# Routing constants made later, and a tile's row copy ahead of the addition to the counts

## The reference, cut

```python
q_pool = q.reshape(B, H, S // 2, 2, D).mean(axis=3)
attn = softmax(scale * q_pool @ k.T)             # scale = 1 / sqrt(D)
x = (attn @ v)                                   # as tokens: N = 2304 rows, 512 columns

# first layer of experts (8 experts, 512 -> 1024 -> 512)
do_compute = x @ w_skip > 0                      # the others keep x
e_idx = argmax(x @ w_gate);  gate_w = probability of that expert
x = x + gate_w * (relu(x @ w1[e_idx]) @ w2[e_idx])

# second layer
e_idx = argmax(x @ w_gate2); gate_w = its probability
eom = sigmoid(x @ w_output_gate)
out = gate_w * eom[e_idx] * (relu(x @ w1b[e_idx]) @ w2b[e_idx])
```

## Time and profile before

| | us |
|---|---|
| median of 3 runs | 1131.06 |
| lowest and highest | 1129.37, 1131.52 |
| the profiled execution | 1127.29 |
| its span, first to last instruction | 1125.5 |
| attention, to the last head's sums | about 549 |
| first layer's tiles | about 571 to 796 |
| change to the second layer | about 796 to 814 |
| second layer | 814 to the end |

### The profile page before, as it was taken

The page is one execution under the profiler, slowest core; times in us unless marked ns, Lnnn a source line. Parts: engine busy times, 40 slices in busy tenths (PEclk is TensorE's granted clock), DMA queues, the critical chain, the costliest instruction groups (busy, mean ns, idle before and its releaser), DMA issues.

```text
span 1125.5 us, 22186 instructions
## 1 busy us (share of the span) xinstructions
PE 1092.2 (97%) x7849; PEld 921.4 (82%) x7849; DVE 741.0 (66%) x1706; ACT 531.8 (47%) x945; POOL 459.0 (41%) x337
## 2 busy tenths in 40 slices
PE   7999999999999999999799999999899999999996
PEld 5777777777777777777598999999799999999995
DVE  7767767887778877786446777777465655566641
ACT  3566655655555665554225444444054344254320
POOL 0768877777876788777600000000000101111100
PEclk9999999999999999999899999999899999999999
DMA  5273225223322233311659014447385281231100
GB/s 132 66 232 75 64 75 149 72 70 95 104 65 74 75 86 96 81 37 33 231 177 354 28 38 179 165 182 277 127 336 175 75 328 37 78 138 40 44 10 15
DMA packets 74398, 132.61 MB, mean 118 GB/s; under 512 B 11040, under 2 KB 29472, under 8 KB 74320
## 3 DMA queue, kind: packets, MB, share of 16 engines
q1 hardware_dynamic: 43568, 50.84, 16.9%
q10 hardware_dynamic: 26096, 68.96, 16.7%
q0 software_dynamic: 4656, 11.79, 3.0%
HBM read 106.12 MB, written 19.24 MB: 111 GB/s over the span
## 4 chain that ended last, share of the span: by engine, by line
PE 94%; DVE 2%; issue 1%; ACTq 1%; ACT 0%; SPq 0%; DMA 0%; POOL 0%; DVEq 0%; POOLq 0%
PE PS L765 24%; PE PS L600 14%; PE PS L514 11%; PE PS L566 9%; PE PS L573 8%; PE PS L583 7%; PE PS L778 6%; PE PS L782 6%; PE PS L779 6%; PE PS L615 1%; PE PS L638 1%; PE PS L797 1%; DVE mx L1070 1%; ACTq L846 0%; DMA moe<-xs 0%
## 5 line engine op out<-in xcount | busy, mean ns | idle before, releaser
L454 POOL TENSOR_TENSOR arena_a<-arena_a,arena_p 128x576 f32<-128x576 f32 x222 | 330.3, 1488 | 85.3 <-ACT arena_p L883 62.7
L1070 DVE TENSOR_REDUCE mx<-PS 128x1 f32<-128x384 f32 (+1 forms) x480 | 246.3, 551 | 108.9 <-PE PS L566 105.3
L765 PE MATMUL PS<-moe,W 128*128 128x128 f32 x2432 | 279.0, 276 | 1.5 <-ACT moe L969 1.5
L765 PEld LDWEIGHTS PS<-moe,W 128*128 128x128 f32 x2432 | 276.2, 192 | 3.7 <-ACT moe L969 1.9
L883 ACT ACTIVATE arena_p<-PS 128x576 f32<-128x576 f32 x288 | 187.6, 653 | 132.0 <-PE PS L583 131.5
L573 PE MATMUL PS<-QHT,KA 128*128 128x288 f32 x576 | 182.0, 329 | 0.0
L1175 DVE TENSOR_TENSOR W2L<-W2R,W2H 128x1024 fp32r<-128x1024 f32 x144 | 169.8, 1220 | 16.4 <-ACT W2H L855 15.9
L566 PE MATMUL PS<-KA,QHT 128*128 128x384 f32 (+1 forms) x480 | 173.7, 364 | 2.2 <-DVE mx L1070 2.0
L583 PE MATMUL PS<-QLT,KB 65*128 65x288 f32 x576 | 171.1, 301 | 0.2 <-ACT QLT L894 0.2
L855 ACT CAST W2H<-W2R 128x1024 fp32r<-128x1024 f32 x148 | 144.3, 1048 | 50.4 <-PE PS L782 41.6
L600 PE MATMUL PS<-arena_p,arena_a 128*64 128x288 f32 x1152 | 160.5, 414 | 0.0
(11 more groups left out here) (181 smaller groups left out, 1154.1 us busy)
## 6 DMA issues: line engine op xcount, KB each, us to landing
W<-in_moe_w ACTq DMA_DIRECT2D x16, 2048.0 KB, 14.9
W2R<-in_moe_w ACTq DMA_DIRECT2D x16, 2048.0 KB, 9.8
moe<-xs SPq DMA_DIRECT2D x40, 258.0 KB, 2.7
arena_a<-in_k SPq DMA_DIRECT2D x32, 288.0 KB, 3.0
arena_a<-in_v SPq DMA_DIRECT2D x32, 288.0 KB, 2.8
KB<-KA SPq DMA_DIRECT2D x32, 288.0 KB, 3.1
arena_a<-in_q SPq DMA_DIRECT2D x32, 256.0 KB, 3.2
xs<-padrow SPq DMA_DIRECT2D x9, 258.0 KB, 3.6
```

What stands on the lines that cost most here:

```text
L454: nc.gpsimd.tensor_tensor(Acc[u], Acc[u], P[u][:, t, :], ALU.add).then_inc(acc_step, 1)
L765: last = nc.tensor.matmul(PS[:, HB + f // 4, (f % 4) * PN:(f % 4 + 1) * PN], W1[s][:, d, f * PN:(f + 1) * PN], xT[:, d, :], start=(d == 0) ...
L1070: vec.reduce_max(mx3[0:n, t, c:c + 1], PS[0:n, MXB + b % 2, 0:KB_], AX.X).then_inc(pr_max, 1)
```

## The change

Two edits, both in the order of VectorE's instructions, and one wait of TensorE. `routing_constants()` stood ahead of VectorE's stage 0; now it stands in stage 1, behind the maximum of prior block 10. TensorE's wait for them moves from ahead of stage 1 to ahead of stage 2. In `tile_route` the addition to the counts and their cast stand behind the row copy and the positions.

```diff
             for h in range(FIRST, LAST):
-                if h == 1:
+                if h == 2:
                     pe.wait_ge(consts_v, 3)
                 body(h)
...
                     route_in(b)
+                    if h == 1 and b == 10:
+                        routing_constants()
...
             for h in range(FIRST, LAST):
-                if h == 0:
-                    routing_constants()
                 body(h)
...
-                then_wait(vec.tensor_tensor(Racc[:, :], Racc[:, :], tR[:, :], ALU.add))
-                vec.tensor_copy(Raccb[:, :], Racc[:, :]).then_inc(rt_acc, 1)
                 dve.wait_ge(os_free, i + 1)
                 vec.tensor_copy(os_, ob).then_inc(os_done, 1)
                 dve.wait_ge(os_done, i + 1)
                 vec.tensor_tensor(tpu[:, :], tpf[:, :], tinv[:, :], ALU.add).then_inc(t_pos, 1)
+                then_wait(vec.tensor_tensor(Racc[:, :], Racc[:, :], tR[:, :], ALU.add))
+                vec.tensor_copy(Raccb[:, :], Racc[:, :]).then_inc(rt_acc, 1)
```

## The result

| | before | after |
|---|---|---|
| median, us | 1132.58 (8 runs) | 1135.87 (8 runs) |
| lowest | 1129.37 | 1134.52 |
| ratio after to before, 95% interval | | 1.0035 [1.0018, 1.0052] |
| profiled execution, span | 1125.5 | 1135.4 |
| mean granted clock in it | 0.992 | 0.985 |

The change makes the kernel some 4 us slower by the ratio. The forecast was +0.83 us and 1131.9, and the range ended at 1134.2: it was wrong in size, and the measured time lies outside. One of the eight executions of before, of 1791.8 us, is far off the others and no part of the ratio.

A forecast was written before the change was run, and what follows sets the result against it. TensorE, 94% busy and full in stage 1, was taken to bound the kernel. The terms 0 + 0.83 + 0 gave +0.83 us on the median of 1131.06, so 1131.9, with a range of 1129.4 to 1134.2.

The forecast's parts named there:

- What bounds the kernel, and where to look: TensorE, 94% busy, bounds the kernel; VectorE's order counts only where TensorE waits; stage 1 is full, stage 0 has air.
- Part 1a: Front of stage 0: taking away VectorE's 1.30 us of constants gains 0, as block 0's maximum waits for TensorE.
- Part 1b: Stage 1 behind block 10: the constants delay block 11's maximum and so TensorE's blocks 13 and 14; loss 0.83 us.
- the sum of 0.83 us: Stage 1: 1.30 us of constants make TensorE's block 14 start at 52.83 instead of 52.00, never given back.
- the lower end: Stage 1: the constants keep their 1.30 us, no cast held; the upper end was a wait to GpSimd's addition's end.
- Rival B: Stage 1: GpSimd's addition holds one cast until it ends; loss 2.2 us, 1133.3, or 1133.8 with the last tile; chance 0.23.
- Rival C: Behind stage 1's wait: TensorE's clock halves for 6.7 us, up to 3.4 us more, 1136.7; chance 0.04.
- Part 2: Routing at the first layer's end: the reordered four instructions still take 0.83 us; cost 0, bounds 0 and +0.54 us.
- the 0.54 us of the full clock: Last routing tile: the counts' cast comes 0.54 us later, paid in full only if TensorE's eight transposes run at full clock.
- the last tile's bound: End of the first layer: up to +0.54 us from the last tile's later cast of the counts; taken as 0.

The follow-up runs named there:

- e4: Against the kernel before: constants made twice, ahead of stage 0 and behind block 10 of stage 1, old routing order; ratio 1.0027, median +3.7 us.
- e6: Against the kernel before: constants behind block 10 with the five casts ahead of the eight memsets, old routing order; ratio 1.0008, median +0.6 us.
- e8: As e6, with three more memsets of 96x384, so VectorE is as late as in the change without a hold; ratio to before 1.0025, median +2.5 us.
- e7: Against the kernel before: only the eight memsets moved behind block 10, casts still ahead of stage 0, old routing order; ratio 1.0004, median -0.5 us.
- e9: The unaltered change measured a third time against the kernel before, on one chip with the move of the constants alone; ratio 1.0030, median +4.1 us.
- e12: The whole change with the five casts ahead of the memsets, new routing order kept, against the kernel before; ratio 1.0015, median +1.9 us.
- e1: Against the kernel before: only the constants moved behind block 10 of stage 1, old routing order; ratio 1.0036, median +3.5 us.
- e5: The unaltered change measured again against the kernel before, beside three variants of the constants; ratio 1.0039, median +3.6 us.

## Why the prediction was wrong, point by point

**What bounds the kernel, and where to look.** Right. The loss sits at the place where TensorE was full and VectorE's idle time was over; nothing gave it back, and the distance between the two traces stays at 6.4 us for thirty heads.

**Part 1a, the front of stage 0 is free.** Right, by e4. The maximum of block 0 waits for TensorE with the constants there or not.

**Part 1b, the sum of 0.83 us.** The chain of the sum held: with 1.34 us of constants (e6) stage 1 grew by 0.85. The step that failed is the price put into it. I took "the lower end" of 1.30 us, on the ground that "an instruction that follows at once on one that got through isn't held". The pair in the earlier trace rows was too thin for that: the held instruction had waited out one addition, and GpSimd's next one, at 308.18, only starts behind both. In the changed kernel the first cast did go ahead, by 0.07 us, and two more behind it, but the fourth was held to the end of the addition. GpSimd itself lost only 0.13 us (1.55 instead of 1.42). The price was 2.52 us instead of 1.30, too low by 1.22, and with it the sum's term is 2.07 us instead of 0.83. Rival B had the loss at 2.2, and named its place and its condition. The rule cited from the Trainium skill (SBUF — State Buffer, "Who interferes with whom") pointed to this result, and the runs agree with it in that five casts are five claims, and one of them waits for the addition's end. They don't agree by reported starts: two casts that start behind the addition still pass. The same section says that a VectorE instruction with at most one SBUF input outside the two-port modes doesn't contend; e8's memsets beside the addition agree.

**Rival C, the clock.** It was B with a fall of the clock on top, at 0.04, and the fall was real in three of seven traces. It was argued away with stage 0's gaps at a full clock. That was one execution's luck: the waits of 0.75 and 0.95 us are there in all fourteen traces, and in four of them the clock falls around the second. The row for it was the 2.22 us at 795.27, behind which the clock is at half in thirteen of fourteen traces (not in e7). Its size was off the other way: a fall behind the wait costs 1.4 us, not 3.4. Since C only needs B and a fall, a good part of B's 0.23 belonged to times above B's 2.2: the kernels with B's wait lost 3.3 us in the mean.

**Part 2.** Right within its bounds. The reordered tile takes the same time, TensorE's wait of 2.22 us is unchanged, and in after L835 comes 3.94 us behind the copy of the logits, against 3.95 before. A part of the 0.54 us of the full clock can be seen too. In e9, at half clock for only a part of the time, TensorE does wait for the cast:

```profile
807.11 0.17 DVE L1305 CAST Raccb<-Racc 128x16 bf16<-128x16 f32 x1
807.34 0.17 PE L835 MATMUL PS<-Raccb,onesb 128*1 128x16 bf16 x1 [0.39 <-DVE Raccb L1305]
```

There it is 3.74 us from the logits to L835 (3.75 in e12), against 3.52 in e1 and e4 with the old order and about the same clock: 0.2 us. With the old order at full clock it is 3.24 in e7. No trace has the new order at full clock there; 3.74 - 3.24 = 0.5 us is an estimate for it. So the new order costs 0, 0.2 or 0.5 us by the state of the clock, below what the medians resolve. A small misreading: the thirty transposes of 3.71 us were not all at full clock, which is 0.94 in 803 to 804.

**The range** ended at 1134.2, just above B's price with the last tile's bound (1133.8). It left out rival C's own case, B with a fall of the clock (1136.7), and the level of before itself moved from 1131.06 to 1132.58 as more runs came in.

## What to carry to other kernels

A small instruction moved beside another engine's long one isn't priced by its old duration: a cast of 32 numbers took 1.37 us here, to the end of GpSimd's addition. So put casts where GpSimd waits, and memsets beside it, as e6 and e8 did. Idle time of an engine is cover only for what stands ahead of its end; the same work one block later is paid in full where TensorE is full. When a rival brings a wait of TensorE of some 2 us, add a share of the clock's price to its own (here up to 1.4 us) instead of keeping it as a separate case of small chance.

## What the runs showed of the hardware

- What passes and what is held doesn't follow the reported starts exactly: two casts that start 0.06 and 0.13 us behind GpSimd's start (54.37) still pass at 0.16 us, and the one at 0.21 us is held. after, e1 and e4 show the same starts and the same 1.37 us.
- A wait of TensorE of 1.85 us was followed by a half clock of some 3.4 us in three of seven traces, from 1.4 to 1.8 us behind its end; one of 3.85 us in the only one taken; one of 2.22 us, at the end of the first layer, in thirteen of fourteen. Those of 0.19 to 0.64 us in stage 1 were followed by none.
- In stage 0 all fourteen traces have the same waits of 0.75 and 0.95 us, and four have a fall of the clock there. It costs more than in stage 2, 2.1 to 2.4 us: in these four TensorE also waits 0.6 to 1.1 us for a maximum some 5 us later, which it doesn't in the others.
- At the end of the attention, ScalarE's L903 comes 2.3 us behind TensorE's second group of L615 in after and in e5 to e8, whatever they change, and 0.9 us in before and all the others. e5 to e8 ran on one chip, but that the chip is the reason isn't shown, and what lies in that 1.4 us wasn't looked into.
